# The gate of an MoE stage kept in the PSUM bank of its product

## Chip, cores and metric

The kernel runs on one core of one Trainium2 chip. The metric is the device time of one execution in microseconds (us). A core has TensorE (PE; PEld is its loading of weights), VectorE (DVE), ScalarE (ACT), GpSimd (POOL) and SyncE (SP, which issues the transfers here). All five run their own instruction queues in order and meet through semaphores.

## Reference

Linear attention with a decay, then two feed-forward stages, all in fp32. Cut to what matters:

```
x = attention(r, k, v, w, u)            # 3072 tokens x 384
h = x @ w_in                            # 384 -> 2048, first stage
g = where(h >= 1, h, where(h <= -1, 0, (h + 1) ** 2 / 4))
x = g @ w_out                           # 2048 -> 384
a = x @ w_gate                          # 384 -> 1536, second stage
out = (a / (1 + exp(-a)) * (x @ w_val)) @ w_out2
```

The piecewise function of the first stage is the "knee"; its result g is the "gate" of this text. The kernel computes it as min(relu(0.5 h + 0.5)^2, max(h, 1)).

## The kernel before

**Blocks and tiles.** The 3072 tokens are taken in NG = 8 blocks of T = 384. In phase 1 each block of the attention's output runs through J1 = 16 hidden tiles of 128 rows; in phase 2 each block runs through J2 = 12. A hidden tile n has number n = 16 g + j. Its product `h` is 128 x 384 in fp32 and fills one PSUM bank, `hid[j % 2]`; `gate`, `ghi` and `glo` are SBUF buffers, also two of each.

**Precision.** Products are made of three fp32r products: every operand is split in a high part (a copy in fp32r) and a low part (operand minus high part). So each gate is split as well: `ghi` by ACT, `glo = gate - ghi` by VectorE.

**One tile of phase 1, in order of dependence** (lines of the kernel before):
- TensorE `tile_in(g, j)` (the products stand at L1168): nine matmuls into `hid[j % 2]`, after a wait that the bank is free (L1175).
- ACT `knee`: relu(0.5 h + 0.5) from the bank into `gate[j % 2]` (L777), and its square in place (L779), after a wait that lo of tile n-2 has been done (L785).
- VectorE `knee` (L1026): min(max(h, 1), gate) from the bank and `gate`, into `gate`.
- ACT `hi` (L770): copies `gate` to `ghi`, once tile_out of tile n-2 is done.
- VectorE `lo` (L1019): `glo = gate - ghi`.
- TensorE `tile_out(1, g, j)` (L1196): nine matmuls with ghi and glo into the three accumulators `acc`.

**Order on the engines.** Each engine has a function `slot(g, j, ...)`, called for all j of all g. TensorE's slot j does tile_in of tile n+2, then attention work for the next block in some slots (`do_fill`; L1214 to L1250), then tile_out of tile n. ACT's does hi of tile n+1 and knee of tile n+2; VectorE's does lo of tile n+1 and knee of tile n+2; then both drain the attention banks, and in some slots do scans (VectorE, L929 and L939, in slots 10, 13 and 14), checks or conversions of weights. In the first block weights of the first stage are still being split (ACT L715, POOL L661, VectorE L1055); at the end of phase 1 those of the second stage are (ACT L871, POOL L661). The last slots of a block already begin the next block's tiles.

**Counters.** `M["g", 1]` counts VectorE's knees and starts with a credit of J1; `M["lo", 1]` counts the lo's, without a credit. `M["q"/"t"/"hi"/"out", ph]` count the other steps. Phase 2 has the same structure with `sig` and `swiglu` in place of the knee; it uses the same `hid`, `gate`, `ghi` and `glo`.

Of the kernel before, what the change touches and what calls it, by code (L numbers as in the profile page):

```python
# [24 lines left out]
F32 = mybir.dt.float32  # L25
F32R = mybir.dt.float32r
U32 = mybir.dt.uint32
ALU = mybir.AluOpType
ACT = mybir.ActivationFunctionType
# [8 lines left out]
T = NW * WIN  # L38
NG = B * S // T
# [3 lines left out]
J1, J2 = FF1 // P, FF2 // P  # L43
# [54 lines left out]
def first(g):  # L98
    return isinstance(g, int) and g == 0
# [10 lines left out]
def build_program(nc, w_d, kr_d, tok_d, u_d, cst_d, w1i_d, w1o_d, w2g_d, w2v_d,  # L110
                  w2o_d, rs_d, ks_d, vs_d, ws_d, us_d, out_d, x2_d, ys_d):
    ctx = ExitStack()
    with ctx:
        at = [nc.sbuf_base + (-nc.sbuf_base) % 32]

        def place(name, shape, dt, offset=None):

            size = 2 if dt == mybir.dt.bfloat16 else 4
            for n in shape[1:]:
                size *= n  # L120
            if offset is None:
                offset = at[0]
                at[0] += (size + 31) // 32 * 32
            assert offset + size <= nc.sbuf_usable_end, (name, offset + size)
            return nc.alloc_sbuf_tensor_at(name, shape, dt, offset=offset), offset + size
# [4 lines left out]
        gate = [place(f"gate{i}", [P, T], F32)[0] for i in range(2)]  # L130
        ghi = [place(f"ghi{i}", [P, T], F32R)[0] for i in range(2)]
        glo = [place(f"glo{i}", [P, T], F32R)[0] for i in range(2)]
# [63 lines left out]
        def w2gv(part, j, gv):  # L196
            return w2a[part][:, j, gv, :] if j < NA else w2b[part][:, j - NA, gv, :]

        bank = [ctx.enter_context(nc.psum_tensor(f"bank{i}", [P, 512], F32)) for i in range(8)]
        hid = bank[0:2]  # L200
        acc = bank[2:5]
        attb = bank[5:8]

        def sem(name):
            return ctx.enter_context(nc.semaphore(name))
# [23 lines left out]
        M = {}  # L229
# [32 lines left out]
        def wait_lo(wait, c):  # L262

            if (c + 1) % DVE_LO == 0:
                wait(wlo_d, (c + 1) // DVE_LO)
            else:
                wait(wlo, c + 1 - (c + 1) // DVE_LO)
# [443 lines left out]
        def _(e):  # L711
# [52 lines left out]
            def hi(ph, g, j):  # L764

                e.wait_ge(M["g", ph], g * J[ph] + (j + 1) + J[ph])
                e.wait_ge(M["out", ph], g * J[ph] + (j - 1) + J[ph])
                if ph == 2 and isinstance(g, int) and g == 0 and j < 2:
                    e.wait_ge(M["out", 1], (NG + 1) * J1 - 1 + j)
                e.activation(ghi[j % 2][:, :], gate[j % 2][:, :], ACT.Copy).then_inc(M["hi", ph], 1)  # L770

            def knee(g, j):

# [49 lines left out]
            more_hi(11)  # L823
            knee(0, 0)
            hi(1, 0, 0)
            knee(0, 1)

# [3 lines left out]
            def slot(g, j, parity, next_half, after_next):  # L831
                last = isinstance(g, int) and g == NG - 1
                finished, started = nxt(g, j + 1, J1), nxt(g, j + 2, J1)
                if not (last and j + 1 >= J1):
                    hi(1, *finished)
                else:
                    hi(2, 0, 0)
                if not (last and j + 2 >= J1):
                    knee(*started)
                else:  # L840
                    sig(0, j + 2 - J1)
                if next_half:
                    for f in WIN_SLOTS.get(j, ()):
                        drain(g + 1, f, 1 - parity)
                if first(g):
                    more_hi(done[0] + 2)
                    if j in CHECK_FIRST:
                        check_w(1, CHECK_FIRST[j])
                if after_next and j in CHECK_SLOTS:
                    check_w(g + 2, CHECK_SLOTS[j])  # L850
                if last and j == 10:
                    split_x(0, 0)
                if last or (g == NG - 2 and j > max(WIN_SLOTS)):

                    for _ in range(2 if last and j > 3 else 1):
                        if w2c[0] < W2_EARLY or j >= J1 - 3:
                            w2_hi(w2c[0])
                            w2c[0] += 1
                if j == J1 - 1:
                    copy_out(1, g)  # L860
# [59 lines left out]
        def _(e):  # L920
# [95 lines left out]

            def lo(ph, g, j):
                e.wait_ge(M["hi", ph], g * J[ph] + (j + 1))
                e.tensor_tensor(glo[j % 2][:, :], gate[j % 2][:, :], ghi[j % 2][:, :].bitcast(F32), ALU.subtract)\  # L1019
                    .then_inc(M["lo", ph], 1)  # L1020

            def knee(g, j):

                e.wait_ge(M["t", 1], g * J1 + (j + 1))
                q = gate[j % 2][:, :]
                e.scalar_tensor_tensor(q, hid[j % 2][:, 0:T], 1.0, q, ALU.max, ALU.min).then_inc(M["g", 1], 1)  # L1026

            def copy_out(ph, g):
                e.wait_ge(M["out", ph], (g + 2) * J[ph])
# [53 lines left out]
            w1_lo(3)  # L1083
            prefix_scan(1, 0)
            knee(0, 0)
            lo(1, 0, 0)
            knee(0, 1)

            def nxt(g, j, J_):
                return (g, j) if j < J_ else (g + 1, j - J_)  # L1090

            def slot(g, j, parity, next_half, after_next):
                last = isinstance(g, int) and g == NG - 1
                if not (last and j + 1 >= J1):
                    lo(1, *nxt(g, j + 1, J1))
                else:
                    lo(2, 0, 0)
                if not (last and j + 2 >= J1):
                    knee(*nxt(g, j + 2, J1))
                else:  # L1100
                    swiglu(0, j + 2 - J1)
# [56 lines left out]
        def _(e):  # L1158
# [3 lines left out]
            def products(out, w_of, x_of, n, start, stop):  # L1162

                total = 3 * n
                i = 0
                for k in range(n):
                    for a, b_ in THREE:
                        m = e.matmul(out, w_of(a, k), x_of(b_, k), start=start and i == 0,  # L1168
                                     stop=stop and i == total - 1)
                        i += 1  # L1170
                return m

            def tile_in(g, j, parity):

                e.wait_ge(M["g", 1], g * J1 + (j - 1) + J1)  # L1175
                if j == 0:
                    e.wait_ge(xl_out, (g + 1) * NW)
                if first(g):
                    wait_lo(e.wait_ge, 2 * j)
                xs = (xhi[parity], xlo[parity])  # L1180
                products(hid[j % 2][:, 0:T], lambda a, k: w1i[a][:, j, k * P:(k + 1) * P],
                         lambda b_, k: xs[b_][:, k, :], KT, True, True).then_inc(M["h", 1], 1)
# [96 lines left out]
            for f in range(NF):  # L1279
                do_fill(0, f, 0)  # L1280
            tile_in(0, 0, 0)
            tile_in(0, 1, 0)

            def tile_in2(g, j, parity):

                e.wait_ge(M["g", 2], g * J2 + (j - 1) + J2)
                if j == 0:
                    e.wait_ge(x2lo, g + 1)
                if isinstance(g, int) and g == 0:
                    e.wait_ge(wlo2, order2.index((j, 1)) + 1)  # L1290
                    if j < 2:
                        e.wait_ge(M["g", 1], NG * J1 + J1 - 1 + j)
                xs = (xhi[parity], xlo[parity])
                for s, out in ((0, hid[j % 2]), (1, attb[j % 2])):
                    m = products(out[:, 0:T], lambda a, k: w2gv(a, j, s)[:, k * P:(k + 1) * P],
                                 lambda b_, k: xs[b_][:, k, :], KT, True, True)
                m.then_inc(M["h", 2], 1)

            def slot(g, j, parity, next_half, after_next):
                last = isinstance(g, int) and g == NG - 1  # L1300
                if j + 2 < J1:
                    tile_in(g, j + 2, parity)
                elif not last:
                    tile_in(g + 1, j + 2 - J1, 1 - parity)
                else:
                    tile_in2(0, j + 2 - J1, 0)
                if last and j == 4:
                    e.wait_ge(w_sum, NG + 2)
                    e.matmul(attb[2][0:1, 0:1], bad[:, OPS_CHECK:OPS_CHECK + 1], ones[:, :], start=True, stop=True).then_inc(w_tot, 1)
                if next_half:  # L1310
                    for f in WIN_SLOTS.get(j, ()):
                        do_fill(g + 1, f, 1 - parity)
                tile_out(1, g, j, w1o)
# [73 lines left out]
```

## Time and profile before

| what | value |
|---|---|
| median of 3 runs | 984.63 us (984.63 to 985.52) |
| the profiled execution | 988.26 us |
| its span, first to last instruction | 986.4 us |
| TensorE busy (matmul) | 961.5 us, 97% of the span |
| VectorE busy | 520.4 us, 53% |
| ACT busy | 404.3 us, 41% |
| POOL busy | 149.6 us, 15% |

A busy TensorE is measured with modelled ends of pipelined matmuls, so that 97% says that it was rarely without an instruction and not that it ran at its peak. The rows in the section below are from the profiled execution; their times count from the start of its span. In the timeline a bracket behind a row gives the idle time of that engine before it and the instruction that is taken to have ended it. Phase 1 ends and phase 2 begins near 530 us.

### The profile page before, as it was taken

What the parts mean: (1) busy time and instruction counts of PE and PEld (TensorE: products, weight loads), DVE (VectorE), ACT (ScalarE), POOL (GpSimd) and SP (SyncE); (2) the same over time, 40 slices, a digit from 0 to 9 for tenths busy, and PEclk for the clock granted to TensorE, in tenths of its full rate; (3) what the DMA queues carried; (4) which work ended last, traced back from release to release, by engine and by line L of the source; (5) the groups of instructions that cost most, each with busy time, mean ns of one, the idle gap of its engine ahead of it and who ended that gap; (6) DMA issues with size and microseconds to landing.
All of it is one profiled execution on the core that took longest, in us unless ns stands there. A gap on an engine that the chain in (4) does not pass through costs nothing.

```text
span 986.4 us, 17455 instructions
## 1 busy us (share of the span) xinstructions
PE 961.5 (97%) x6874; PEld 942.9 (96%) x6874; DVE 520.4 (53%) x913; ACT 404.3 (41%) x849; POOL 149.6 (15%) x146
## 2 busy tenths in 40 slices
PE   5898999999999999999999999999999999999998
PEld 4788999999999999999999999999999999999997
DVE  7795757666566675675434443434334334434332
ACT  5755546445454554554575322222222222222222
POOL 6582120210202103020253400000000000000000
PEclk9998999999999999999999999999999999999999
DMA  8816131312212122200332201010100101010000
GB/s 244 275 44 165 58 96 44 96 56 74 83 57 80 61 86 58 82 26 1 113 105 85 85 1 49 1 49 1 49 0 0 48 0 48 0 48 0 24 1 26
DMA packets 23493, 59.52 MB, mean 60 GB/s; under 512 B 2689, under 2 KB 12033, under 8 KB 23425
## 3 DMA queue, kind: packets, MB, share of 16 engines
q1 hardware_dynamic: 23424, 58.59, 18.8%
q8 instruction: 46, 0.75, 0.3%
q14 instruction: 23, 0.18, 0.1%
HBM read 49.14 MB, written 9.44 MB: 59 GB/s over the span
## 4 chain that ended last, share of the span: by engine, by line
PE 91%; DVE 3%; DMA 2%; issue 1%; ACT 1%; SPq 0%; POOL 0%; DVEq 0%; ACTq 0%
PE bank L1168 48%; PE bank L1196 34%; PE bank L1222 3%; PE bank L1244 2%; PE bank L1239 2%; PE bank L1250 1%; PE bank L1214 1%; PE bank L1231 1%; DMA r_k_v_by_token<-in_rkv_token 1%; DMA ring<-in_w_gate 1%; DVE glo L1019 1%; DVE gate L1026 0%; DVE suf L929 0%; DVE state_decayed L980 0%; DMA ring<-in_w_out 0%
## 5 line engine op out<-in xcount | busy, mean ns | idle before, releaser
L770 ACT ACTIVATE ghi<-gate 128x384 fp32r<-128x384 f32 x224 | 117.2, 523 | 190.6 <-DVE gate L1038 95.4
L1019 DVE TENSOR_TENSOR glo<-gate,ghi 128x384 fp32r<-128x384 f32 x224 | 133.0, 594 | 114.8 <-ACT ghi L770 112.4
L1036 DVE TENSOR_TENSOR gate<-bank,gate 128x384 f32<-128x384 f32 x96 | 53.5, 558 | 215.0 <-ACT gate L889 215.0
L1168 PE MATMUL bank<-xhi,w2gv_ahi 128*128 128x384 f32 x480 | 161.3, 336 | 0.0
L1168 PE MATMUL bank<-xlo,w2gv_ahi 128*128 128x384 f32 x480 | 161.3, 336 | 0.0
L1168 PE MATMUL bank<-xhi,w2gv_alo 128*128 128x384 f32 x480 | 161.3, 336 | 0.0
L889 ACT ACTIVATE gate<-bank 128x384 f32<-128x384 f32 x96 | 47.2, 492 | 227.7 <-PE bank L1168 227.7
L1196 PE MATMUL bank<-ghi,w1ohi 128*128 128x384 f32 x384 | 134.5, 350 | 0.7 <-DVE glo L1019 0.7
L1168 PE MATMUL bank<-xhi,w1ihi 128*128 128x384 f32 x384 | 129.5, 337 | 5.0 <-DVE gate L1026 2.3
L1196 PE MATMUL bank<-glo,w1ohi 128*128 128x384 f32 x384 | 129.7, 338 | 0.0
L1196 PE MATMUL bank<-ghi,w1olo 128*128 128x384 f32 x384 | 129.6, 337 | 0.0
L1168 PE MATMUL bank<-xhi,w1ilo 128*128 128x384 f32 x384 | 129.3, 337 | 0.0
L1168 PE MATMUL bank<-xlo,w1ihi 128*128 128x384 f32 x384 | 129.2, 337 | 0.0
L1026 DVE SCALAR_TENSOR_TENSOR gate<-bank,gate 128x384 f32<-128x384 f32 x128 | 71.2, 556 | 107.5 <-ACT gate L779 107.4
L777 ACT ACTIVATE gate<-bank 128x384 f32<-128x384 f32 x128 | 62.7, 490 | 90.4 <-PE bank L1168 88.4
L1196 PE MATMUL bank<-ghi,w2ohi 128*128 128x384 f32 x288 | 96.8, 336 | 0.0
L1196 PE MATMUL bank<-ghi,w2olo 128*128 128x384 f32 x288 | 96.8, 336 | 0.0
L1196 PE MATMUL bank<-glo,w2ohi 128*128 128x384 f32 x288 | 96.8, 336 | 0.0
L1168 PEld LDWEIGHTS bank<-xhi,w2gv_ahi 128*128 128x128 f32 x480 | 90.2, 188 | 0.0
L1168 PEld LDWEIGHTS bank<-xlo,w2gv_ahi 128*128 128x128 f32 x480 | 90.2, 188 | 0.0
L1168 PEld LDWEIGHTS bank<-xhi,w2gv_alo 128*128 128x128 f32 x480 | 90.2, 188 | 0.0
L1168 PEld LDWEIGHTS bank<-xhi,w1ihi 128*128 128x128 f32 x384 | 72.5, 189 | 5.9 <-issue 3.3
(93 smaller groups left out, 1532.0 us busy)
## 6 DMA issues: line engine op xcount, KB each, us to landing
r_k_v_by_token<-in_rkv_token SPq DMA_DIRECT2D x24, 576.0 KB, 5.3
k_r_by_channel<-in_kr_channel SPq DMA_DIRECT2D x24, 448.0 KB, 4.1
w_by_channel<-in_w_channel SPq DMA_DIRECT2D x24, 226.2 KB, 2.7
x_t<-ring SPq DMA_DIRECT2D x8, 576.0 KB, 3.0
x_raw<-x_t SPq DMA_DIRECT2D x8, 576.0 KB, 4.0
ring<-in_w_out SPq DMA_DIRECT2D x22, 192.0 KB, 3.4
out_t<-ring SPq DMA_DIRECT2D x7, 576.0 KB, 3.1
ring<-in_w_gate SPq DMA_DIRECT2D x12, 192.0 KB, 2.3
```

The lines of the kernel that those rows point to most:

```text
L770: e.activation(ghi[j % 2][:, :], gate[j % 2][:, :], ACT.Copy).then_inc(M["hi", ph], 1)
L777: e.activation(q, hid[j % 2][:, 0:T], ACT.Relu, bias=0.5, scale=0.5).then_inc(M["q", 1], 1)
L889: e.activation(gate[j % 2][:, :], hid[j % 2][:, 0:T], ACT.Sigmoid).then_inc(M["q", 2], 1)
L1019: e.tensor_tensor(glo[j % 2][:, :], gate[j % 2][:, :], ghi[j % 2][:, :].bitcast(F32), ALU.subtract)\
L1026: e.scalar_tensor_tensor(q, hid[j % 2][:, 0:T], 1.0, q, ALU.max, ALU.min).then_inc(M["g", 1], 1)
L1036: e.tensor_tensor(q, hid[j % 2][:, 0:T], q, ALU.mult).then_inc(M["t", 2], 1)
L1168: m = e.matmul(out, w_of(a, k), x_of(b_, k), start=start and i == 0, stop=stop and i == total - 1)
L1196: m = e.matmul(acc[k][:, 0:T], wo[a][:, j, k * P:(k + 1) * P], gs[b_][:, :], start=(j == 0 and i == 0), stop=(j == J[ph] - 1 and i == 2))
L1214: m = e.transpose(out[:, p * PR:(p + 1) * PR], kr[:, w, 0, p, :], ident[0:PR, 0:PR])
L1222: m = e.matmul(o[:, p * WIN:(p + 1) * WIN], kr[r, w, 0, p, :], kr[r, w, 1, p, :], start=True, stop=True)
L1239: e.matmul(out[t, p * 2 * D:(p + 1) * 2 * D], kr[:, w, 1, p, t], sbar[twin(g, w)][:, p, :], start=(p == 0), stop=False, skip_group_check=True)
L1244: m = e.matmul(out[t, h * D:(h + 1) * D], att[twin(g, w)][h % 2][:, h // 2, t], tok[:, w, 2, h * D:(h + 1) * D], start=(row_start and h == 0),
```

## The change

VectorE's knee writes its result into `hid[j % 2]`, over the product that it reads, instead of into `gate`. In phase 1 `hi` and `lo` then take the gate from that bank; in phase 2 they read the SBUF buffer as before. ACT's two steps still write `gate`. Since the bank now holds the gate until both have read it, TensorE's tile_in of tile n waits for lo of tile n-2 instead of VectorE's knee of tile n-2; the first two tiles wait for none. The first two tiles of phase 2 wait for the last two lo's of phase 1.

```diff
+        def gate_of(ph, j):
+
+            return hid[j % 2][:, 0:T] if ph == 1 else gate[j % 2][:, :]
...
-                e.activation(ghi[j % 2][:, :], gate[j % 2][:, :], ACT.Copy).then_inc(M["hi", ph], 1)
+                e.activation(ghi[j % 2][:, :], gate_of(ph, j), ACT.Copy).then_inc(M["hi", ph], 1)
...
-                e.tensor_tensor(glo[j % 2][:, :], gate[j % 2][:, :], ghi[j % 2][:, :].bitcast(F32), ALU.subtract)\
+                e.tensor_tensor(glo[j % 2][:, :], gate_of(ph, j), ghi[j % 2][:, :].bitcast(F32), ALU.subtract)\
                     .then_inc(M["lo", ph], 1)
...
                 e.wait_ge(M["t", 1], g * J1 + (j + 1))
-                q = gate[j % 2][:, :]
-                e.scalar_tensor_tensor(q, hid[j % 2][:, 0:T], 1.0, q, ALU.max, ALU.min).then_inc(M["g", 1], 1)
+                h = hid[j % 2][:, 0:T]
+                e.scalar_tensor_tensor(h, h, 1.0, gate[j % 2][:, :], ALU.max, ALU.min).then_inc(M["g", 1], 1)
...
-                e.wait_ge(M["g", 1], g * J1 + (j - 1) + J1)
+                if g * J1 + j - 1 > 0:
+                    e.wait_ge(M["lo", 1], g * J1 + (j - 1))
...
-                        e.wait_ge(M["g", 1], NG * J1 + J1 - 1 + j)
+                        e.wait_ge(M["lo", 1], NG * J1 - 1 + j)
```

## Rows read from the trace of the kernel before

**Rows 1.** The page, part 2: TensorE's granted clock in tenths, 40 slices.

```profile
PEclk9998999999999999999999999999999999999999
```

**Rows 2.** Busy time by stretch (start:end, length, PE, PEld, DVE, ACT, POOL, clock, DMA, GB/s).

```profile
29.60:108.60 79.00, 70.18 (x572) 67.03 (x572) 62.66 (x98) 48.19 (x111) 36.65 (x31) 0.96 0.47 135
...
108.60:170.90 62.30, 62.30 (x535) 60.31 (x534) 40.19 (x76) 31.99 (x69) 9.41 (x9) 1.00 0.22 72
```

**Rows 3.** Groups of instructions by line, shapes kept apart: busy us, mean ns, idle before.

```profile
L1019 DVE TENSOR_TENSOR glo<-gate,ghi 128x384 fp32r<-128x384 f32 x224 | 133.0, 594 | 114.8 <-ACT ghi L770 112.4
...
L1026 DVE SCALAR_TENSOR_TENSOR gate<-bank,gate 128x384 f32<-128x384 f32 x128 | 71.2, 556 | 107.5 <-ACT gate L779 107.4
...
L1014 DVE TENSOR_TENSOR xlo<-bank,xhi 128x384 fp32r<-128x384 f32 x24 | 13.0, 543 | 1.7 <-ACT xhi L761 1.7
...
L761 ACT ACTIVATE xhi<-bank 128x384 fp32r<-128x384 f32 x24 | 11.7, 487 | 12.8 <-PE bank L1250 12.8
```

**Rows 4.** Timeline at the first turn: start us, length, engine, line, instruction.

```profile
106.24 0.55 DVE L1026 SCALAR_TENSOR_TENSOR gate<-bank,gate 128x384 f32<-128x384 f32 x1
...
108.25 1.23 DVE L939 TENSOR_TENSOR_SCAN w_by_channel<-w_by_channel,scan_seed 112x516 f32<-112x516 f32 x1
...
108.98 0.19 PEld L1168 LDWEIGHTS bank<-xhi,w1ihi 128*128 128x128 f32 x1
...
109.46 0.55 DVE L1019 TENSOR_TENSOR glo<-gate,ghi 128x384 fp32r<-128x384 f32 x1
...
111.07 0.56 DVE L1019 TENSOR_TENSOR glo<-gate,ghi 128x384 fp32r<-128x384 f32 x1
...
112.10 0.19 PEld L1168 LDWEIGHTS bank<-xhi,w1ihi 128*128 128x128 f32 x1
```

**Rows 5.** Timeline at the turn from the sixth block to the seventh.

```profile
421.19 0.19 PEld L1168 LDWEIGHTS bank<-xhi,w1ihi 128*128 128x128 f32 x1
...
421.68 0.55 DVE L1019 TENSOR_TENSOR glo<-gate,ghi 128x384 fp32r<-128x384 f32 x1
```

**Rows 6.** Timeline at the turn from the seventh block to the eighth.

```profile
480.72 0.19 PEld L1168 LDWEIGHTS bank<-xhi,w1ihi 128*128 128x128 f32 x1
...
481.22 0.53 ACT L871 ACTIVATE w2gv_ahi<-ring 128x384 fp32r<-128x384 f32 x1 [3.77 <-DMA ring<-in_w_gate]
...
482.19 1.06 DVE L1019 TENSOR_TENSOR glo<-gate,ghi 128x384 fp32r<-128x384 f32 x1 [4.15 <-ACT ghi L770]
...
483.31 0.45 PE L1196 MATMUL bank<-ghi,w1ohi 128*128 128x384 f32 x1 [0.69 <-DVE glo L1019]
```

**Rows 7.** Timeline of the first block: TensorE, POOL and VectorE.

```profile
37.70 0.44 PE L1168 MATMUL bank<-xhi,w1ihi 128*128 128x384 f32 x1 [2.26 <-DVE gate L1026]
...
37.81 1.02 POOL L661 TENSOR_TENSOR w1olo<-ring_b,w1ohi 128x384 fp32r<-128x384 f32 x1
...
38.24 1.00 DVE L1019 TENSOR_TENSOR glo<-gate,ghi 128x384 fp32r<-128x384 f32 x1 [0.59 <-ACT ghi L770]
...
47.05 0.19 PEld L1168 LDWEIGHTS bank<-xhi,w1ihi 128*128 128x128 f32 x1
...
48.42 0.55 DVE L1019 TENSOR_TENSOR glo<-gate,ghi 128x384 fp32r<-128x384 f32 x1
...
56.83 0.41 PE L1168 MATMUL bank<-xhi,w1ihi 128*128 128x384 f32 x1 [1.44 <-POOL w1ilo L661]
...
65.40 0.46 PE L1222 MATMUL bank<-k_r_by_channel 48*128 48x128 f32 x3 [0.90 <-DVE x_by_token L1011]
...
71.40 0.19 PEld L1168 LDWEIGHTS bank<-xhi,w1ihi 128*128 128x128 f32 x1
...
72.10 1.08 DVE L1019 TENSOR_TENSOR glo<-gate,ghi 128x384 fp32r<-128x384 f32 x1
...
82.04 2.08 PE L1222 MATMUL bank<-k_r_by_channel 48*128 48x128 f32 x16 [2.87 <-DVE x_by_token L1011]
```

**Rows 8.** Busy time by stretch: the dip of the clock (0.50).

```profile
81.70:88.50 6.80, 6.46 (x31) 6.27 (x32) 3.86 (x9) 3.68 (x9) 2.20 (x3) 0.50 0.99 257
```

## Prediction, made before the changed kernel was run

> **What bounds the kernel now.** I read the page first: TensorE's granted clock is down only near 85 us, by the tenths of part 2 [rows 1]. Then busy time by stretch, one row for each pass over a block of 384 tokens: from the second block on TensorE is busy for the whole stretch (62.30 of 62.30 us) while VectorE has 40.19 and ACT 31.99; only the first block leaves it idle (70.18 of 79.00) [rows 2]. So faster VectorE or ACT instructions are worth nothing by themselves outside the first block, and every microsecond for which a new wait stops TensorE is lost. The question of this case is the slack of one wait. I therefore went through the timeline tile by tile and asked, for each of the 128 hidden tiles of the first stage: at what time does TensorE start the product `tile_in` of tile n+2, and at what time has VectorE ended `lo` of tile n?
>
> The cycle of one tile is: TensorE `tile_in(n)` into `hid[n%2]`; ACT's two steps of the knee; VectorE's `knee`; ACT's `hi`; VectorE's `lo`; TensorE `tile_out(n)`. TensorE's order is tile_in(n+2), some attention work in some slots, tile_out(n).
>
> **What the change adds: a longer hold of the bank.** Before, tile_in(n+2) waits for `knee(n)`, the last reader of `hid[n%2]`. After, the gate lies in that bank until `lo(n)` has read it, so tile_in(n+2) waits for lo(n), two instructions later (ACT `hi`, VectorE `lo`). tile_out(n) waited for lo(n) anyway, but tile_in(n+2) was the 1.6 us of work that hid it. Queued behind this wait on TensorE are the attention work of the slot, tile_out(n) and all that follows. Where lo(n) ends before tile_in(n+2) would start, the price is nothing; where it is late, the price is the lateness plus about 0.05 us of signalling. In most slots of the steady blocks lo(n) is early enough, the least of them being the lo at 111.07, which ends at 111.63, 0.47 before its tile_in at 112.10 [rows 4]: no cost, and the cover is the rest of the cycle (tile_out and tile_in of the neighbours, the attention work). It is late in three places.
>
> *The turn from one block to the next.* VectorE has two scans queued between knee and lo. At the first turn: knee at 106.24, a scan that starts at 108.25 as the last of its pair, then lo at 109.46 to 110.01, while the tile_in that now must wait for it begins to load weights at 108.98 [rows 4]. It would start at 110.01 + 0.05 = 110.06: 1.08 us late. (The tile before it is late too, by less, but this lo does not depend on that product, being held by the scans, so the delays do not add: the turn costs the larger of the two.) At the turn from the sixth block to the seventh the same pair stands at 421.19 and 421.68 + 0.55: again 1.04 + 0.05 [rows 5]. The pattern stands at six turns: 6 x 1.08 = 6.5 us. Nothing behind it has idle time that could take this up, since TensorE is busy throughout [rows 2].
>
> *The turn from the seventh block to the eighth.* There ACT sits in a conversion of a second-stage weight whose transfer lands late (3.77 us of idle time), so `hi` and with it `lo` come late: lo runs from 482.19 to 483.25, and tile_in began at 480.72 [rows 6]. This lo took 1.06 us where 0.55 is usual; with one operand in PSUM I expect 0.55 (below), so it ends at 482.74 and tile_in starts at 482.79, 2.07 late. In exchange the stall that stood here behind tile_in, before the first tile_out product at 483.31, goes: 0.69 us is given back. Net +1.4.
>
> *The first block.* TensorE is stopped here already, by 2.26 us before tile_in at 37.70, 1.44 at 56.83 (a weight's low half from POOL), 0.90 at 65.40 and 2.87 at 82.04 (a bank that VectorE drains; that drain stands behind weight work whose transfer is late) [rows 7]. New stops fall between: lo at 38.24 would end at 38.79, so that tile_in starts 1.1 us later than 37.70. VectorE loses some 0.5 by it, as its next knee follows that product through ACT. The lo at 48.42 then ends at about 49.5, and the tile_in of 47.05 starts 2.5 us late. The stalls at 56.83 and 65.40 are set by POOL and VectorE, not by TensorE, and take back 1.44 + 0.90 = 2.3. The lo at 72.10 ends at 72.65 and makes the tile_in of 71.40 late by 1.3; the 2.87 at 82.04 takes that back. At the end of these the first block is where it was, or a little ahead, because VectorE's own chain has grown shorter by the 0.5 us of a slow lo at a time; I put down -0.4.
>
> **What it makes faster or slower.** (a) `lo`, 128 of 224 instances, now reads PSUM and SBUF where it read SBUF twice. Mean 594 ns before, against 543 ns for the same subtraction `xlo` with one operand in PSUM [rows 3]. Its bad cases are 1.00, 1.08 and 1.06 us [rows 6, 7]; the first lies beside a POOL instruction on two SBUF operands, from 37.81 for 1.02 us [rows 7]. The mean of 543 leaves no room for such cases among the instances of `xlo`. I take 0.55. The Trainium skill, page SBUF — State Buffer, section "SBUF: two separate sides", says VectorE with two SBUF inputs and GpSimd exclude each other for a whole instruction; by that rule the slow cases go, the trace agrees. (b) `hi` reads PSUM: 487 ns as `xhi` [rows 3]; it is off the path. (c) `knee` writes PSUM instead of SBUF. No VectorE instruction of this trace writes PSUM. Bounds: 487 ns (an ACT instruction of this size) and 594 ns (the slowest mean of this size on VectorE) against 556 [rows 3]; I keep 556. Per turn a difference of that size enters once, so -0.4 to +0.2 us over six turns.
> Against the change speaks the Trainium skill, page VectorE: DVE Perf Modes, section on the TRN2 errata: a PSUM source costs 120 fixed cycles on VectorE where an SBUF source costs 58, an estimate of 0.065 us more for each lo. By it the sum would be 0.4 us higher. Rows 3 say the opposite (543 against 594), so I leave it out.
> (d) The number of waits of TensorE is unchanged, no DMA is touched, and the second stage keeps its code but for two waits at its start that were met long before.
>
> **The sum.** 6.5 + 1.4 - 0.4 = +7.5 us. On the profiled execution (988.26, of which the span is 986.4) that gives 995.8; on the median of the runs shown, 984.63, which is 3.6 below the profiled one, it gives 992.1.
>
> **The clock.** After the 2.87 us of idle time the clock stood at 0.50 (1.2 GHz) from 81.7 to 88.5 us [rows 7, 8]. TensorE was busy for 6.46 us of them, so that half of it, 3.2 us, is what the dip cost. By my own account the idle time at 82.04 shrinks to about 1, so this loss may go; but the idle time before 37.70 grows from 2.26 (which left the clock at 2.4 GHz) to 3.4 us, which may bring one there, where later stalls absorb half. I do not know whether the unprofiled runs hold the dip at all. I let the two stand against each other.
>
> **Rivals.**
> 1. *The clock's dip goes and none replaces it:* 992.1 - 3.2 = 988.9. For it: the shorter idle time at 82.04. Against it: the longer one at 37.70.
> 2. *A further dip or slower PSUM writes:* a stop of about 2.1 us at 480.72 or of 3.4 at 37.70 brings the clock down for as long as at 81.7, on a stretch where TensorE has no slack: 6.8 / 2 = 3.4 us, 995.5. The 2.26 that left it up speaks against the one, nothing against the other.
> 3. *Not slower:* POOL and VectorE exclude each other in the first block more than I allow. The place is the first block, the mechanism the freed operand: if the slow lo's (about 0.5 us each, five of them from 38.24 to 72.10) and POOL's own waits come out of one chain, the three stalls 1.44, 0.90 and 2.87 go with the dip: 5.2 + 3.2 = 8.4 against 6.5 + 1.4 = 7.9 added, 984.1. It decides once VectorE's chain is more than 2.5 us ahead at 82.04; against it speaks that its drain waits there for a transfer that the change does not touch.
> 4. *The new wait does not bind at the turns:* the counts could be met earlier than I read them, with the effect gone: 984.6. The counts are plain (tile n waits for n-1 lo's), so this is small.
>
> **Chances.** Forecast 0.52, rival 1 0.22, rival 2 0.18, rival 3 0.05, rival 4 0.03. The range that holds 8 in 10 runs from 988.5, just below rival 1, to 995.9, just above rival 2; it holds the bounds of (c) and of the skill's figure. What can be told from no change is 0.2%, 2.0 us: of rivals 3 and 4 I give 0.02 to faster, 0.06 to same, the rest is slower.
>
> **What the profile after would show.** At each of six turns an idle stretch of TensorE before a tile_in, in two pieces of 0.5 to 0.6 us, released by VectorE `lo`; before 482.8 (plus the shift) one of 2 us; blocks two to six longer by about 1.1 us each. lo in the first stage at 0.53 to 0.56 us without outliers; hi near 0.49; knee near 0.56. I would be wrong if the turns show no stop; if the first block ends more than 3 us earlier or later than before; or if products themselves grow slower while VectorE or ACT holds the other bank of `hid`, which no row here suggests.

## The result, and the profile after

| what | before | after |
|---|---|---|
| median of 4 runs each | 984.82 us | 991.13 us (990.36 to 992.37) |
| ratio to before | 1 | 1.0064, 95% interval 1.0047 to 1.0081 |
| profiled execution, span | 988.26, 986.4 us | 990.36, 988.6 us |

The changed kernel is 6.3 us slower; 7.5 had been forecast. The two profiled executions lie only 2.2 us apart in span, and a good part of what follows is about why. First the page of the changed kernel, whose lines answer to the granted clock and the groups of [rows 1, 3], with the busy times:

```profile
PE 963.2 (97%) x6874; PEld 940.0 (95%) x6874; DVE 514.8 (52%) x913; ACT 400.5 (41%) x849; POOL 139.3 (14%) x146
...
PEclk9999999999999999999999999999999999999999
...
L1172 PE MATMUL bank<-xhi,w1ihi 128*128 128x384 f32 x384 | 131.3, 342 | 9.7 <-DVE glo L1023 8.3
...
L1030 DVE SCALAR_TENSOR_TENSOR bank<-bank,gate 128x384 f32<-128x384 f32 x128 | 72.2, 564 | 121.6 <-ACT gate L783 121.5
...
L1023 DVE TENSOR_TENSOR glo<-bank,ghi 128x384 fp32r<-128x384 f32 x128 | 70.5, 551 | 56.9 <-ACT ghi L774 55.6
...
L774 ACT ACTIVATE ghi<-bank 128x384 fp32r<-128x384 f32 x128 | 62.3, 487 | 89.5 <-PE bank L1201 53.5
```

VectorE, ACT and POOL all have less work, and the kernel is slower. What grew is the idle time of TensorE in front of `tile_in` (L1172): 9.7 us, of which 8.3 ended with VectorE's `lo`. The wait list of TensorE names it as a wait that was not there before (waiter, releaser, total, times, longest):

```profile
PE bank L1172 <- DVE glo L1023: 8.3, 17, 2.5
```

Seventeen stops: four in the first block, two at each of six turns, one at the last turn. The first turn in the timeline, to be held against [rows 4]:

```profile
100.84 0.53 DVE L1023 TENSOR_TENSOR glo<-bank,ghi 128x384 fp32r<-128x384 f32 x1
...
101.43 0.45 PE L1172 MATMUL bank<-xhi,w1ihi 128*128 128x384 f32 x1 [0.19 <-DVE glo L1023]
...
103.30 1.23 DVE L943 TENSOR_TENSOR_SCAN w_by_channel<-w_by_channel,scan_seed 112x516 f32<-112x516 f32 x1
...
104.50 0.55 DVE L1023 TENSOR_TENSOR glo<-bank,ghi 128x384 fp32r<-128x384 f32 x1
...
105.11 0.44 PE L1172 MATMUL bank<-xhi,w1ihi 128*128 128x384 f32 x1 [0.23 <-DVE glo L1023]
```

Each `tile_in` starts 0.06 us after a `lo` ends (104.50 + 0.55 = 105.05, 105.11). The bracket of 0.23 us understates the loss, because the modelled end of the matmul before (0.34 us long) reaches far behind the time at which the next could have been issued (they start 0.17 us apart in these rows). The loss is read from starts. The last of the six turns, to be held against [rows 5]:

```profile
422.15 0.55 DVE L1023 TENSOR_TENSOR glo<-bank,ghi 128x384 fp32r<-128x384 f32 x1
...
422.76 0.45 PE L1172 MATMUL bank<-xhi,w1ihi 128*128 128x384 f32 x1 [0.29 <-DVE glo L1023]
```

From the third `tile_in` of the second block to that of the seventh it took 421.19 - 108.98 = 312.21 us before [rows 4, 5] and takes 422.76 - 105.11 = 317.65 now: 5.44 for five turns, 1.09 each on average. They are not alike. At each of them the two stops add 0.52 and 0.56 us, and 0.07 comes back with the next tile, because the second load of weights after a stop follows the first by 0.11 us instead of 0.17: 1.02 in all. Behind the second, fourth and sixth turn three tiles take 3.18 us where 3.12 is usual, 0.18 more; no stop shows there. From the first `tile_in` of the second block to that of the eighth the six turns come to 6.6 us (374.86 us before, 381.50 now; these begin at 102.74 and 477.60, and at 97.79 and 479.29). The turn from block seven to eight, to be held against [rows 6] (the first two rows are ACT's conversion that stands waiting for its transfer, and hi behind it; the third is POOL's split of the same weight, beside lo):

```profile
482.71 0.52 ACT L875 ACTIVATE w2gv_ahi<-ring 128x384 fp32r<-128x384 f32 x1 [3.57 <-DMA ring<-in_w_gate]
...
483.14 0.47 ACT L774 ACTIVATE ghi<-bank 128x384 fp32r<-128x384 f32 x1
...
483.31 0.99 POOL L665 TENSOR_TENSOR w2gv_alo<-ring,w2gv_ahi 128x384 fp32r<-128x384 f32 x1 [27.57 <-ACT w2gv_ahi L875]
...
483.65 0.56 DVE L1023 TENSOR_TENSOR glo<-bank,ghi 128x384 fp32r<-128x384 f32 x1 [3.90 <-ACT ghi L774]
...
484.26 0.44 PE L1172 MATMUL bank<-xhi,w1ihi 128*128 128x384 f32 x1 [1.52 <-DVE glo L1023]
```

And the first block, to be held against [rows 7]: the stop before the third tile_in, those that lo causes further on, and the place of the former 2.87 us:

```profile
38.44 0.45 PE L1172 MATMUL bank<-xhi,w1ihi 128*128 128x384 f32 x1 [2.55 <-DVE glo L1023]
...
49.13 0.44 PE L1172 MATMUL bank<-xhi,w1ihi 128*128 128x384 f32 x1 [0.77 <-DVE glo L1023]
...
57.64 0.44 PE L1172 MATMUL bank<-xhi,w1ihi 128*128 128x384 f32 x1 [0.31 <-DVE glo L1023]
...
72.26 0.44 PE L1172 MATMUL bank<-xhi,w1ihi 128*128 128x384 f32 x1 [0.54 <-DVE glo L1023]
...
80.07 0.49 PE L1227 MATMUL bank<-k_r_by_channel 48*128 48x128 f32 x4
```

The last row has no bracket: the stop of 2.87 us is gone, and the third tile of the second block starts 108.98 - 105.11 = 3.87 us earlier than before, although a turn of 1.09 lies in front of it. So the first block alone is 4.95 us shorter in these two executions (the first `tile_in` of the second block begins to load its weights at 97.79 instead of 102.74), which is also outside the 3 us that the prediction named as a sign of being wrong:

```profile
102.74 0.19 PEld L1168 LDWEIGHTS bank<-xhi,w1ihi 128*128 128x128 f32 x1
```

```profile
97.79 0.19 PEld L1172 LDWEIGHTS bank<-xhi,w1ihi 128*128 128x128 f32 x1
```

The stretch at half clock of [rows 8] is not there either:

```profile
81.70:88.50 6.80, 6.80 (x51) 6.55 (x51) 5.37 (x11) 6.58 (x17) 3.48 (x3) 1.00 0.96 241
```

TensorE issued 51 matmuls in it where 31 had gone before. Together: -4.95 in the first block, +6.6 at six turns, +0.8 at the last, which is +2.4 at the end of phase 1; the spans differ by 2.2.

### The profile page after: what moved, and what is told of

Same layout as the page of the kernel before. It is cut to its first block, busy times and chain, and to the rows that moved or that the text cites. A ratio compares the mean times of both kernels' runs of the same rounds, so it can differ in the third digit from the quotient of the medians.

```text
span 988.6 us, 17454 instructions
## 1 busy us (share of the span) xinstructions
PE 963.2 (97%) x6874; PEld 940.0 (95%) x6874; DVE 514.8 (52%) x913; ACT 400.5 (41%) x849; POOL 139.3 (14%) x146
## 4 chain that ended last, share of the span: by engine, by line
PE 89%; DVE 6%; issue 2%; ACT 2%; DMA 1%; POOL 0%; DVEq 0%; SPq 0%; ACTq 0%; POOLq 0%
PE bank L1172 48%; PE bank L1201 31%; PE bank L1227 3%; PE bank L1249 2%; DVE suf L933 2%; PE bank L1244 2%; PE bank L1219 1%; PE bank L1255 1%; PE bank L1236 1%; DVE w_by_channel L943 1%; DVE glo L1023 1%; DMA ring<-in_w_gate 1%; DVE bank L1030 0%; ACT gate L783 0%; DVE k_r_by_channel L955 0%
## 5 line engine op out<-in xcount | busy, mean ns | idle before, releaser
L1172 PE MATMUL bank<-xhi,w2gv_alo 128*128 128x384 f32 x480 | 161.3, 336 | 0.0
L1172 PE MATMUL bank<-xhi,w2gv_ahi 128*128 128x384 f32 x480 | 161.3, 336 | 0.0
L1172 PE MATMUL bank<-xlo,w2gv_ahi 128*128 128x384 f32 x480 | 161.3, 336 | 0.0
L1172 PE MATMUL bank<-xhi,w1ihi 128*128 128x384 f32 x384 | 131.3, 342 | 9.7 <-DVE glo L1023 8.3
L1030 DVE SCALAR_TENSOR_TENSOR bank<-bank,gate 128x384 f32<-128x384 f32 x128 | 72.2, 564 | 121.6 <-ACT gate L783 121.5
L1172 PE MATMUL bank<-xhi,w1ilo 128*128 128x384 f32 x384 | 129.3, 337 | 0.0
L1172 PE MATMUL bank<-xlo,w1ihi 128*128 128x384 f32 x384 | 129.2, 336 | 0.0
L1023 DVE TENSOR_TENSOR glo<-bank,ghi 128x384 fp32r<-128x384 f32 x128 | 70.5, 551 | 56.9 <-ACT ghi L774 55.6
L774 ACT ACTIVATE ghi<-bank 128x384 fp32r<-128x384 f32 x128 | 62.3, 487 | 89.5 <-PE bank L1201 53.5
L1201 PE MATMUL bank<-ghi,w2olo 128*128 128x384 f32 x288 | 96.8, 336 | 0.0
L1201 PE MATMUL bank<-glo,w2ohi 128*128 128x384 f32 x288 | 96.8, 336 | 0.0
L1172 PEld LDWEIGHTS bank<-xlo,w2gv_ahi 128*128 128x128 f32 x480 | 90.3, 188 | 0.0
L1172 PEld LDWEIGHTS bank<-xhi,w2gv_alo 128*128 128x128 f32 x480 | 90.3, 188 | 0.0
L1172 PEld LDWEIGHTS bank<-xhi,w2gv_ahi 128*128 128x128 f32 x480 | 90.3, 188 | 0.0
L774 ACT ACTIVATE ghi<-gate 128x384 fp32r<-128x384 f32 x96 | 50.4, 525 | 95.3 <-DVE gate L1042 95.3
```

The costliest lines, as they stand in the source:

```text
L774: e.activation(ghi[j % 2][:, :], gate_of(ph, j), ACT.Copy).then_inc(M["hi", ph], 1)
L1023: e.tensor_tensor(glo[j % 2][:, :], gate_of(ph, j), ghi[j % 2][:, :].bitcast(F32), ALU.subtract)\
L1030: e.scalar_tensor_tensor(h, h, 1.0, gate[j % 2][:, :], ALU.max, ALU.min).then_inc(M["g", 1], 1)
L1201: m = e.matmul(acc[k][:, 0:T], wo[a][:, j, k * P:(k + 1) * P], gs[b_][:, :], start=(j == 0 and i == 0), stop=(j == J[ph] - 1 and i == 2))
```

## Experiments

All medians and ratios below are against the kernel before, run on the same chip in the same rounds. Its executions spread from 982.8 to 989.1 us there (70 runs in three sessions, medians 985.88, 986.26 and 986.29), so ratios are compared, not microseconds of different sessions; 0.001 is 1 us.

**1. The wait alone.** The kernel before with nothing but the new wait of `tile_in`:

```diff
-                e.wait_ge(M["g", 1], g * J1 + (j - 1) + J1)
+                if g * J1 + j - 1 > 0:
+                    e.wait_ge(M["lo", 1], g * J1 + (j - 1))
...
-                        e.wait_ge(M["g", 1], NG * J1 + J1 - 1 + j)
+                        e.wait_ge(M["lo", 1], NG * J1 - 1 + j)
```

> The kernel before with one thing of the change: tile_in of tile n waits for lo of tile n-2. The gate stays in SBUF, lo still reads SBUF twice. My theory (the whole loss is TensorE waiting for lo): six turns at 1.08 us = 6.5; at the turn from block seven to eight lo keeps its slow 1.06 us, so the tile_in is 2.6 late and 0.7 comes back, +1.9; the first block keeps its slow lo's and gives nothing back, 0 to +1.5. In all +8.4 to +9.9, that is 993 to 995 us, 2 to 4 us slower than the changed kernel, which is what the PSUM operand gives back. Rival (the operands in PSUM are what costs: matmuls or VectorE slowed by traffic on the banks): as before, 984.8.

Measured 995.54 us, ratio 1.0093 (1.0077 to 1.0109), +9.2 us, within the +8.4 to +9.9 of the expectation. Its waits of TensorE (waiter, releaser, total, times, longest) have this line:

```profile
PE bank L1168 <- DVE glo L1019: 11.8, 18, 3.9
```

and its `lo` reads in the view of one line's instructions (minimum, median and maximum in ns):

```profile
L1019 DVE TENSOR_TENSOR glo<-gate,ghi x224: 527/558/1375, 38.8 to 987.7; 128x384 fp32r<-128x384 f32 x112
```

The wait with all operands where they were costs more than the whole change does. So the loss is the wait, and no traffic on the banks is needed for it. The changed kernel's `lo` in the same view:

```profile
L1023 DVE TENSOR_TENSOR glo<-bank,ghi x128: 525/556/559, 37.8 to 532.4; 128x384 fp32r<-128x384 f32 x128
...
L1023 DVE TENSOR_TENSOR glo<-gate,ghi x96: 551/558/1119, 537.1 to 981.7; 128x384 fp32r<-128x384 f32 x96
```

The median is the same, 556 and 558 ns; only the outliers went, from 1375 to 559. The two kernels are 2.9 us apart (0.0029). In the profiles they part in the first block, by 5.75 us (the second block begins at 103.54 here and at 97.79 in the changed kernel), of which about 3 are a stretch at half clock that only experiment 1's profile holds. That the remaining 2.9 us come from the outliers is argued; the section on the prediction comes back to it.

**2. The scans cut apart.** The changed kernel with each pair of scans spread over two slots:

```diff
-SCAN_SLOTS = {10: 0, 13: 1, 14: 2}
+SUFFIX_SLOTS = {10: 0, 12: 1, 14: 2}
+PREFIX_SLOTS = {11: 0, 13: 1, 15: 2}
...
-                    if j in SCAN_SLOTS:
-                        scan_window(g + 2, SCAN_SLOTS[j])
+                    if j in SUFFIX_SLOTS:
+                        suffix_scan(g + 2, SUFFIX_SLOTS[j])
+                    if j in PREFIX_SLOTS:
+                        prefix_scan(g + 2, PREFIX_SLOTS[j])
```

> The changed kernel with VectorE's three pairs of scans for the block after next each cut in two: the suffix scan in slots 10, 12 and 14 and the prefix scan in slots 11, 13 and 15, so that no slot has two scans between a knee and its lo. My theory: lo of the first tile of a block comes 1.2 us earlier, the stops at the six turns go, 6.5 us less than the changed kernel, about 984.6. Rival (the stops would only move to other slots, or the loss is not in the turns): 988 to 991.

Measured 985.60 us, ratio 0.9997 (0.9986 to 1.0008). The 6.4 us of the change are gone, and from the first `tile_in` of the second block to the third of the seventh it takes 318.45 us, as in the kernel before. Its TensorE waits for lo fell from 17 to 5, as its list of waits shows:

```profile
PE bank L1175 <- DVE glo L1024: 5.9, 5, 3.4
```

and in its timeline `lo` lies ahead of the tile_in that needs it at the first turn:

```profile
104.05 0.55 DVE L1024 TENSOR_TENSOR glo<-bank,ghi 128x384 fp32r<-128x384 f32 x1
...
105.39 0.19 PEld L1175 LDWEIGHTS bank<-xhi,w1ihi 128*128 128x128 f32 x1
```

lo ends at 104.60, 0.79 us before the weights of tile_in begin to load. No stop moved to another slot of these blocks.

**3. ACT's conversion later.** The changed kernel; in the seventh block ACT converts its first second-stage weight in slot 15, not from slot 13 on:

```diff
-                if last or (g == NG - 2 and j > max(WIN_SLOTS)):
+                if last or (g == NG - 2 and j == J1 - 1):
```

> The changed kernel, but in the seventh block ACT converts the first second-stage weight in slot 15 instead of slots 13 to 15, so that it does not stand waiting for the transfer in front of hi. My theory: the stop of 1.5 us in the turn from block seven to eight goes, 1.5 to 2.2 us less than the changed kernel, 989 to 989.7. Rival (the stop moves behind the next conversion or into phase 2, whose weights come later): no difference, 991.

Measured 988.43 us, ratio 1.0031 (1.0019 to 1.0042), 3.3 less than the changed kernel by the ratios (the intervals allow 0.5 to 6). In the profiles the second tile_in of the eighth block starts at 481.25 (weights) where the changed kernel has 484.26, and 1.16 of these 3.01 us lie ahead of the turn: the turn gives 1.85, which was within the 1.5 to 2.2 expected. The stop did not move on; TensorE waits for lo 16 times, not 17.

**4. A longer hold, first attempt.** The changed kernel with one more VectorE instruction, whose result nobody reads, between knee and lo at each of the six turns; its buffer `spare` stands ahead of the weights:

```diff
+        spare, _ = place("spare", [P, 1], F32)
...
+                if after_next and j == SUM_SLOT:
+                    e.wait_ge(ld["u"], 16)
+                    e.tensor_reduce(spare[:, :], uu[:, :], AX.X, ALU.add)
```

> The changed kernel with one more VectorE instruction (a sum over 128x384 in SBUF, 0.54 us, its result unused) at each of the six turns, between the knee and the lo of the first tile of the next block. My theory: each turn is longer by the time from one start to the next of such an instruction, 0.47 us, so 6 x 0.47 = 2.8 us more than the changed kernel, 994. Rival (TensorE is not held by lo there): no difference.

Measured 1004.50 us, ratio 1.0188 (1.0170 to 1.0207): 12.4 more than the changed kernel, where 2.8 had been expected. The second tile of each turn did grow by 0.46 us (4.14 instead of 3.68), but every tile of both phases had become longer as well, by 0.05 to 0.06 us, also far from any turn. The four bytes of `spare` had pushed all weights and the buffers behind them 32 bytes further. That made two questions of one, and experiments 5 and 11 take them apart.

**5. The same, at unchanged addresses.** `spare` now stands behind all other buffers.

> The changed kernel with the same additional VectorE instruction at each of the six turns as in the run before, but with its 4-byte result behind all other buffers in SBUF, so that no buffer lies at another address than in the changed kernel. My theory (TensorE is held by lo at the turns): each turn 0.47 us longer, 2.8 us more than the changed kernel; and the slowing of every tile by 0.05 us that the run before showed was the 32 bytes by which its buffers had moved, and is gone. Rival (any additional VectorE work costs 13 us): as the run before.

Measured 996.24 us, ratio 1.0100 (1.0076 to 1.0123). The slowing of each tile is gone. At the first turn:

```profile
111.37 0.55 DVE L1133 TENSOR_REDUCE spare<-u_rows 128x1 f32<-128x384 f32 x1
...
111.83 0.55 DVE L1024 TENSOR_TENSOR glo<-bank,ghi 128x384 fp32r<-128x384 f32 x1
...
112.43 0.44 PE L1176 MATMUL bank<-xhi,w1ihi 128*128 128x384 f32 x1 [0.74 <-DVE glo L1024]
```

The idle time is 0.74 where the changed kernel has 0.23, and the two tiles of each of the six turns take 0.46 us longer than in the changed kernel (7.78 instead of 7.32 at the first), as the starts of VectorE's instructions, 0.46 apart, ask for: 2.8 us. Over the whole stretch of the six turns the profiles differ by 2.2, because the tiles of 3.18 us behind every other turn of the changed kernel's profile are not in this one. The medians differ by 3.6 by the ratios (the intervals allow about 1 to 6). This profile holds 10.2 us at half clock and the changed kernel's none (below); how much of the difference of the medians that is, isn't shown.

**6. The same additional instruction in the kernel before.**

> The kernel before with the same additional VectorE instruction at the same six places, its result behind all other buffers. My theory: here lo is late as well, but tile_in runs in the meantime and ends 1.1 us after lo would, so that 0.47 us more is hidden: no difference to the kernel before. Rival (VectorE's work costs at the turns in either kernel): 2.8 us more.

Measured 987.05 us, ratio 1.0011 (0.9999 to 1.0024). The turns are unchanged to 0.01 us: the distance of the third tile_in of the second block to that of the seventh, five turns, is 420.50 - 108.29 = 312.21 us, the same as in [rows 4, 5], although lo now ends 1.5 us behind the start of that tile_in:

```profile
108.29 0.19 PEld L1172 LDWEIGHTS bank<-xhi,w1ihi 128*128 128x128 f32 x1
...
108.77 0.55 DVE L1129 TENSOR_REDUCE spare<-u_rows 128x1 f32<-128x384 f32 x1
...
109.24 0.55 DVE L1020 TENSOR_TENSOR glo<-gate,ghi 128x384 fp32r<-128x384 f32 x1
```

Experiments 5 and 6 are the case in one pair: the same 0.46 us of VectorE's work costs 0.46 us at every turn with the new wait and nothing with the old one.

**7 and 8. Both repairs, on the changed kernel and on the kernel before.** The edits of experiments 2 and 3 together.

> The changed kernel with both repairs: the pairs of scans cut in two over neighbouring slots, and ACT's first second-stage conversion in slot 15 of the seventh block. My theory: the two savings add, 5.5 + 2.5 = 8 us less than the changed kernel, 983. It is then faster than the kernel before by what the PSUM operand gives in the first block. Rival (they take up the same time): 985.

> The kernel before with the same two repairs (pairs of scans cut in two, ACT's first second-stage conversion in slot 15). What it tells: how much of the gain of the repaired changed kernel is owed to the gate in PSUM. My theory: here the turns never stopped TensorE, so cutting the scans gives nothing, and the late conversion gives the 0.7 to 0.9 us of the stop before tile_out; 0.5 to 1 us less than the kernel before, about 985.3, that is 1.5 us more than the repaired changed kernel, whose first block is earlier. Rival (the repairs help both alike): the same as the repaired changed kernel, 983.8.

Measured: changed kernel with both 983.76 us, ratio 0.9979 (0.9964 to 0.9994), that is 8.4 us below the changed kernel and 2.1 below the kernel before; kernel before with both 985.35 us, 0.9989 (0.9980 to 0.9998). On the kernel before the late conversion gives 1.0 us at the last turn of the profile, and the cut scans nothing at the others. The two differ by 1.0 us in favour of the gate in PSUM, but their intervals overlap, so this is not settled.

**9 and 10. The first tile's lo earlier.** Both repairs, and in the first block:

```diff
             suffix_scan(1, 0)
-            w1_lo(3)
-            prefix_scan(1, 0)
             knee(0, 0)
+            w1_lo(3)
             lo(1, 0, 0)
+            prefix_scan(1, 0)
             knee(0, 1)
```

> As the run before it (changed kernel, both repairs), and in the first block VectorE does knee and lo of the first tile ahead of a prefix scan of 2 us that stood in front of both. TensorE's stop of 2.5 to 3.4 us before its third tile_in shrinks by some 2 us. My theory: 1 to 2 us less than with both repairs alone, as part of it is lost again where VectorE sets the pace, about 981.5. Rival (VectorE sets the pace of the whole first block): the same as with both repairs.

> The kernel before with both repairs and with VectorE's first knee and lo ahead of a prefix scan in the first block, the pair to the fastest version of the changed kernel (982.5). My theory: its tile_in waited for the knee alone, so the earlier knee gives TensorE's stop of 2.3 us back in part; but VectorE and the weight chain set the pace behind it: 0 to 1 us less than with the repairs alone, 984.5, still 1.5 to 2 us behind the changed kernel's version. Rival (the gate in PSUM brings nothing in the first block): the same as that version.

Measured: on the changed kernel 982.49 us, ratio 0.9975 (0.9959 to 0.9992), the fastest version of this study; on the kernel before 984.40 us, 0.9983 (0.9971 to 0.9995). The stop before the third tile_in shrank from 2.61 to 1.29 us in the changed kernel's profile, and by the end of the first block nothing of it was left (+0.18 us): VectorE and the weights set the pace of that block, as the rival said. In the medians neither differs from its pair without this edit by more than the intervals allow. Again the changed kernel's version is ahead by 0.8 us, and again that is within the intervals.

**11. Only the addresses.** The kernel before with the unused buffer of experiment 4 and no other difference.

> The kernel before with an unused 4-byte buffer placed ahead of the weights, which moves all weights and everything behind them by 32 bytes in SBUF; no instruction differs. My theory (from the run in which every tile became 0.05 us longer): 96 second-stage tiles at 0.06 and 128 first-stage tiles at 0.05, 5.8 + 6.4 = 12 us more at most, 994 to 998 us, with the time from start to start of some matmuls at 182 instead of 174 ns. Rival (it was the additional instruction): no difference.

Measured 999.37 us, ratio 1.0128 (1.0105 to 1.0150): 12.6 us. Between 700 and 900 us TensorE is busy throughout in both kernels, but issues fewer matmuls; first the kernel before, then this one:

```profile
700.00:900.00 200.00, 200.00 (x1156) 200.00 (x1155) 77.42 (x136) 49.93 (x97) 0.00 (x0) 1.00 0.07 24
```

```profile
700.00:900.00 200.00, 200.00 (x1138) 200.00 (x1138) 76.44 (x134) 48.91 (x95) 0.00 (x0) 1.00 0.07 24
```

1156 against 1138 is 1.6% of TensorE's rate, with nothing but an address between them. The 999.37 us lie above the 994 to 998 expected. This is what experiment 4 had mixed into its result.

## Why the prediction was right, and where it was not

**The six turns: right.** Expected 1.08 us each, 6.5 in all; measured 1.09 on average and 6.6 in all. That the numbers agree so closely is partly luck: the two stops take the 1.08 expected, but 0.07 of it comes back, and the 0.18 behind every other turn had not been foreseen. The prediction named products that grow slower as a sign against it; these tiles of 3.18 us are a small case of it, 0.6 us in all, with no cause found (the kernel before has none, and the profile of experiment 5 has none either). That the delays of two successive tiles do not add, since the second lo is held by the scans, held as well: the first tile is 0.52 us late and the second brings it to 1.08. Experiments 1, 2, 5 and 6 show the mechanism from four sides: the wait without the operands, the operands without late lo's, a longer hold with and without the wait.

**The last turn: right in kind, the size 0.6 us too large.** Expected +1.4, measured +0.8. The lateness was 1.85, not 2.07. The larger part is what is given back. I had put down the 0.69 us in the bracket of [rows 6]; the shift of the tiles shows that it fell from 3.54 to 2.45 us behind the stop, so 1.09 came back. The bracket counts from a modelled end, as at the turns above, and a stop is longer than its bracket. With one operand in PSUM lo took 0.56, as expected, although a POOL instruction runs beside it just as before (from 483.31 for 0.99 us here, from 481.82 for 1.01 in the kernel before).

**The shorter instructions: right.** lo 551 ns (0.55 was taken), hi 487 (487), knee into PSUM 564 (556). The step that spoke against the change, a PSUM source costing VectorE some 0.065 us more (the Trainium skill, page VectorE: DVE Perf Modes, section on the TRN2 errata), has nothing in the rows: medians of 556 ns with one operand in PSUM and 558 with none. What was rightly seen is the lock between VectorE and GpSimd (the Trainium skill, page SBUF — State Buffer, "SBUF: two separate sides"): of 128 lo's not one took over 559 ns once the second SBUF operand was gone. The trace agrees: in the first stage of the kernel before 18 of 128 lo's took more than 0.6 us, and all 18 overlap a POOL instruction; in the changed kernel 42 overlap one and none is slow. The worst cases in the first block, 1.18 and 1.28 us (at 62.10 and 65.33), were larger than the 1.00 to 1.08 that the prediction listed.

**The first block: wrong in size.** The step reads "a bank that VectorE drains; that drain stands behind weight work whose transfer is late", and from it I took 2.87 us of cover that the change could not move, and in rival 3 "its drain waits there for a transfer that the change does not touch". The transfer isn't touched, but its issue waits for VectorE. These rows, before and after, are a scaling on VectorE, the next load on SP's queue, which by the code waits for that scaling, and ACT's conversion of the weight that comes behind it in the queue:

```profile
74.34 1.49 DVE L954 TENSOR_TENSOR k_r_by_channel<-k_r_by_channel,w_by_channel 112x512 f32<-112x512 f32 x1
...
75.86 0.31 SPq L536 DMA_DIRECT2D w_by_channel<-in_w_channel  x1
...
79.71 0.52 ACT L715 ACTIVATE w1ohi<-ring 128x384 fp32r<-128x384 f32 x1 [3.10 <-DMA ring<-in_w_out]
```

```profile
73.21 1.31 DVE L958 TENSOR_TENSOR k_r_by_channel<-k_r_by_channel,w_by_channel 112x512 f32<-112x512 f32 x1
...
74.55 0.31 SPq L540 DMA_DIRECT2D w_by_channel<-in_w_channel  x1
...
77.73 0.53 ACT L719 ACTIVATE w1ohi<-ring 128x384 fp32r<-128x384 f32 x1 [0.34 <-DMA ring<-in_w_out]
```

VectorE is 1.3 us ahead when it ends the scaling (75.83, 74.52), the issue follows by 0.03 us in both, the conversion is 2.0 us ahead (where the other 0.7 come from isn't shown), and TensorE begins the work behind the freed bank at 80.07 instead of 82.04. The stops there take the new waits up and close. So of the 4.95 us of the block 2.0 stand at this restart, where I had 0.4, and 3.0 follow between it and the fifteenth `tile_in` (14.13 us before, 11.15 after), where the clock is the difference; the prediction's estimate was 3.2.

The other profiles let the two causes be told apart by an estimate: the start of the second block's first `tile_in`, less half of the time at half clock before it.

| profile | start | at half clock | start less half of it |
|---|---|---|---|
| kernel before | 102.74 | 6.8 | 99.3 |
| experiments 6 and 8 (old wait, operands in SBUF) | 102.05, 100.41 | 6.8, 3.4 | 98.6, 98.7 |
| experiment 1 (new wait, operands in SBUF) | 103.54 | 6.8 | 100.1 |
| changed kernel | 97.79 | 0 | 97.8 |
| experiments 2, 3 and 7 (new wait, gate in PSUM) | 99.15, 96.75, 97.10 | 3.4, 0, 0 | 97.4, 96.8, 97.1 |
| experiment 5 (the same, with the additional instruction) | 104.65 | 10.2 | 99.5 |

By this the new wait alone costs the first block about 1 us, the gate in PSUM gives back 2 to 3, and together the block gains some 1.6, where -0.4 had been put down. Experiment 5 does not fit (its stop of 2.59 us before 85.37 is there again), so it holds for eight of these nine profiles. That the gain comes from the slow lo's, 2.8 us over their usual length in five of them up to 72.10 in the kernel before, agrees with experiment 1, where they are still slow (1.29 us at 69.64, for one) and the same scaling ends only at 80.1 us.

**The clock: the rival was partly the case.** I had left open whether runs without the profile hold the dip. The mean granted clock, recorded for every run, is never above 0.998 in 70 runs of the kernel before. In the four runs of the changed kernel it is 0.999, 0.998, 0.997 and 1.000, and in experiment 3 it is 0.999 or 1.000 in six of seven. So the dip is mostly there before and often not after. The forecast put this gain at nothing, and rival 1 (988.9) took it in full with 3.2 us. The profiled execution of the kernel before (988.26 us at 0.996, against a median of 984.82) held a dip of 6.8 us; half of the 70 runs have 0.998, and the profiles of experiments 8 and 10, also at 0.998, hold one of 3.4, which costs 1.7 by the same estimate.

**The sum.** With all terms as measured in the two profiles it is 6.6 + 0.8 - 2.0 - 3.0 = +2.4. With 1.6 for the first block and without the clock it is 6.6 + 0.8 - 1.6 = +5.8, and with the clock of a typical run between +4.1 and +5.8. The medians have +6.3, and the interval of the ratio allows 4.6 to 8.0. So the forecast of +7.5 was right in its largest term and gave too little credit in the others: 0.6 us at the last turn, about 1.2 in the first block, and the clock. Had the pair of profiles been the measure, it would have been 5 us off; that the medians are closer is owed in part to the kernel before holding less of the dip in most runs than in the one that was profiled, and that is luck.

## What to carry to other kernels

A buffer that is reused is held until its last reader; before moving an intermediate result into it, list by tile how long before the next writer that reader ends, and look at the turns of the outer loop, where other work is queued between, not at the mean slot. If it is late there, the repair is to split what stands between (here pairs of scans, 6.6 us by the ratios for six new lines). Repair the kernel before as well, to see what the change itself is worth: here both repairs bring the changed kernel to 0.9979 and the kernel before to 0.9989, and the intervals overlap. And when an experiment adds a buffer, put it behind all others, so that no other address changes.

## What the runs showed of the hardware

**Addresses in SBUF.** Moving all weights and the buffers behind them by 32 bytes, with not one instruction changed, cost 1.28% (1.05 to 1.50). The matmuls that had started every 173 to 174 ns then started up to 182 ns apart in part of the cases, the mean of a second-stage tile going from 4.68 to 4.75 us. By the kernel's order of buffers `xhi`, `xlo`, `ghi` and `glo`, the data that TensorE multiplies with the weights, lie ahead of the unused one and kept their addresses, so of the operands of the two feed-forward stages only the weights moved. Whether their own address counts or their distance to the other operand, and which steps are good, wasn't tried. Steps of 179 ns also stand in the slow tiles behind every other turn of the changed kernel, where no address had changed, so addresses aren't the only cause of them.

**When the clock fell.** The profiles show the stretches at 0.50 (1.2 GHz) and the idle time of TensorE ahead of them. The stop before the third tile_in: 2.55, 2.61 and 2.61 us (changed kernel, experiments 3 and 7) left the clock up; 3.35, 3.39, 3.41 and 3.86 us (experiments 2, 4, 5 and 1) were each followed by 3.4 or 6.8 us at half clock, but so was one of 2.22 (experiment 11), while 2.26 was not [rows 1, 7]. At 56 to 57 us one of 2.08 (experiment 6) was followed by 3.4 us at half clock, one of 2.09 (experiment 10) by none. The stop near 80 us: 2.59 to 3.30 us in the kernel before and experiments 5, 6, 8, 10 and 11, each followed by a dip; at most 0.3 in the others, none with a dip there. So stops between 2 and 3 us went either way in these profiles. That is part of the spread of the runs: in experiment 1 the five order by the mean clock, from 992.94 us at 0.999 to 997.66 at 0.996, but in experiment 10 the fastest run (981.81) has 0.997 and one of 986.22 has 0.998, and the 35 runs of the kernel before at 0.998 alone lie between 983.7 and 986.9. The costliest such stretch, after the 3.86 us stop of experiment 1:

```profile
39.80 0.69 PE L1168 MATMUL bank<-xhi,w1ihi 128*128 128x384 f32 x1 [3.86 <-DVE glo L1019]
```

```profile
38.60:45.40 6.80, 5.59 (x17) 5.60 (x18) 3.28 (x6) 3.84 (x10) 2.38 (x3) 0.50 0.81 268
```
